# A linear-attention round in a new order: next k turned beside the scores, outputs in the middle, state at the end

## The reference

```python
for t in range(S):
    cur = np.einsum('bhd,bhe->bhde', u[None] * kt, vt)
    y[:, :, t] = np.einsum('bhd,bhde->bhe', rt, state + cur)
    state = wt[:, :, :, None] * state + np.einsum('bhd,bhe->bhde', kt, vt)
```

## Time and profile before

| | us |
|---|---|
| median of 3 runs | 448.57 |
| lowest and highest of them | 442.07, 450.49 |
| the profiled execution | 442.72 |
| its span in the trace | 441.2 |
| TensorE busy | 409.9 (93%) |
| VectorE busy | 215.4 (49%) |
| GpSimd busy | 167.2 (38%) |
| ScalarE busy | 110.5 (25%) |

### The profile page before, as it was taken

The page is one execution under the profiler, slowest core; times in us unless marked ns, Lnnn a source line. Parts: engine busy times, 40 slices in busy tenths (PEclk is TensorE's granted clock), DMA queues, the critical chain, the costliest instruction groups (busy, mean ns, idle before and its releaser), DMA issues.

```text
span 441.2 us, 6924 instructions
## 1 busy us (share of the span) xinstructions
PE 409.9 (93%) x2682; PEld 394.6 (89%) x2682; DVE 215.4 (49%) x416; ACT 110.5 (25%) x218; POOL 167.2 (38%) x174
## 2 busy tenths in 40 slices
PE   5459898798998999999999999999999999999997
PEld 5448787687888989998999999999999999999997
DVE  4077788679876985623165365635013203212311
ACT  3244244334451110204730021224013103201300
POOL 6173647445424783434769999200000000000000
PEclk9957699789999999999999999999999999999999
DMA  9965443244442310020021233000010000000000
GB/s 141 273 121 124 104 106 84 41 104 99 117 91 36 91 37 0 1 73 0 2 72 37 72 107 108 3 0 1 18 37 0 19 18 19 2 36 18 1 19 36
DMA packets 60130, 25.04 MB, mean 57 GB/s; under 512 B 51136, under 2 KB 58176, under 8 KB 60096
## 3 DMA queue, kind: packets, MB, share of 16 engines
q1 hardware_dynamic: 60096, 24.58, 23.8%
HBM read 22.22 MB, written 2.36 MB: 56 GB/s over the span
## 4 chain that ended last, share of the span: by engine, by line
PE 77%; DVE 10%; issue 6%; SPq 3%; POOL 2%; DMA 2%; ACT 0%; DVEq 0%; POOLq 0%
PE bank L1020 21%; PE bank L1022 21%; PE bank L1021 21%; PE bank L1107 5%; PE bank L1103 2%; DVE suf L796 2%; DVE pre L805 2%; DVE am L829 2%; DMA ub<-in_u 2%; PE bank L1070 2%; SPq L332 1%; PE bank L1140 1%; PE bank L1158 1%; PE bank L1034 1%; POOL rp L525 1%
## 5 line engine op out<-in xcount | busy, mean ns | idle before, releaser
L716 ACT ACTIVATE ha_hi<-bank 128x384 fp32r<-128x384 f32 x48 | 23.6, 492 | 113.1 <-PE bank L1022 113.1
L941 DVE SCALAR_TENSOR_TENSOR ha_lo<-bank,ha_hi 128x384 fp32r<-128x384 f32 x48 | 26.8, 558 | 50.2 <-ACT ha_hi L716 50.2
L1020 PE MATMUL bank<-c_hi,ha_lo 128*128 128x384 f32 x144 | 48.2, 335 | 0.0
L1022 PE MATMUL bank<-c_hi,ha_hi 128*128 128x384 f32 x144 | 48.1, 334 | 0.0
L1022 PE MATMUL bank<-u2T_hi,c_hi 128*128 128x384 f32 x144 | 48.1, 334 | 0.0
L1021 PE MATMUL bank<-c_lo,ha_hi 128*128 128x384 f32 x144 | 48.1, 334 | 0.0
L1020 PE MATMUL bank<-u2T_hi,c_lo 128*128 128x384 f32 x144 | 48.1, 334 | 0.0
L1021 PE MATMUL bank<-u2T_lo,c_hi 128*128 128x384 f32 x144 | 48.1, 334 | 0.0
L946 DVE TENSOR_TENSOR x<-bank,x 128x384 f32<-128x384 f32 x12 | 6.7, 558 | 65.3 <-PE bank L1022 65.3
L1020 PE MATMUL bank<-sg_hi,z_lo 128*128 128x384 f32 x96 | 32.7, 341 | 1.9 <-issue 1.3
L525 POOL TENSOR_TENSOR rp<-rT,pre 112x512 f32<-112x512 f32 x12 | 15.3, 1277 | 46.6 <-ACT rT L648 41.5
(11 more groups left out here) (142 smaller groups left out, 938.1 us busy)
## 6 DMA issues: line engine op xcount, KB each, us to landing
raw<-in_moe_w_ch SPq DMA_DIRECT2D x12, 384.0 KB, 3.1
kc<-in_k SPq DMA_DIRECT2D x12, 192.0 KB, 3.2
rc<-in_r SPq DMA_DIRECT2D x12, 192.0 KB, 3.6
vn<-in_v SPq DMA_DIRECT2D x12, 192.0 KB, 2.9
raw<-in_moe_w_sg SPq DMA_DIRECT2D x6, 384.0 KB, 4.2
out<-x SPq DMA_DIRECT2D x12, 192.0 KB, 1.9
raw<-in_moe_w_in SPq DMA_DIRECT2D x4, 384.0 KB, 6.2
raw<-in_moe_w_tok SPq DMA_DIRECT2D x4, 384.0 KB, 3.4
```

The costliest lines, as they stand in the source:

```text
L716: sc.activation(ha[0][:, i, :], bank[:, 0:HALF], ACT.Relu).then_inc(act_out, 1)
L941: ve.scalar_tensor_tensor(ha[1][:, i, :], bank[:, 0:HALF], 0.0, ha[0][:, i, :].bitcast(F32), ALU.max, ALU.subtract).then_inc(dve_out, 1)
L1020: te.matmul(dst, left[1], right[0], start=first, stop=False)
L1022: return te.matmul(dst, left[0], right[0], start=False, stop=last)
```

## The change

The rounds are put in another order on TensorE and VectorE, and the jobs are dealt anew to the slots.

- TensorE: turn_w(1) stands ahead of the first scores. In a round: scores, kp turned, next k turned, slot 0, next r turned, outputs, w of n + 2 turned, range sum (round 2), slot 1, state products, slot 2. The next k waits for the state sum of the round before, the state products for the next round's kp. Eight calls of the filler matmul go (`keep_busy(4)` in slot 1 of rounds 0 and 1).
- VectorE: decays of n + 1, masks, slot 0, k scaled for n + 1, y and x of the same round, slot 1, state, diagonal of n + 1, slot 2. `st` is made by four `tensor_scalar`, one for each pair of heads, in place of one `tensor_tensor`. The range is marked and counted in round 2.
- ScalarE: the state is copied behind the jobs of slot 2, and the range checks are spread over rounds 0 and 1.
- GpSimd: the products of round 1, a weight split and chunk 2 without its `diagonal_v` come ahead of the branch. The splits of `w_out` are a round later.
- SyncE: k(1) and u are issued ahead of v(0) and r(1). v waits for the state products too. Some weight pieces come a round later.

```diff
 SLOT = {
-    (2, 2): [("xT", 0, 0), ("xT", 0, 1)],
-    (3, 0): [("v", 0, 0)], (3, 1): [("xT", 0, 2)], (3, 2): [("v", 0, 1)],
-    (4, 0): [("v", 0, 2)], (4, 1): [("xT", 0, 3)], (4, 2): [("u", 0, 0), ("wsg", 0, 0), ("wsg", 0, 1)],
-    (5, 0): [("v", 0, 3)], (5, 1): [("xT", 0, 4)], (5, 2): [("u", 0, 2), ("wsg", 0, 2), ("wsg", 0, 3)],
-    (6, 0): [("v", 0, 4)], (6, 1): [("xT", 0, 5), ("u", 0, 4)], (6, 2): [("wsg", 0, i) for i in range(4, 8)],
-    (7, 0): [("v", 0, 5)], (7, 1): [("u", 0, 6), ("u", 0, 1)], (7, 2): [("wsg", 0, 8), ("u", 0, 3), ("wsg", 0, 9)],
-    (8, 0): [("u", 0, 5), ("wsg", 0, 10)], (8, 1): [("u", 0, 7), ("wsg", 0, 11)], (8, 2): [("sg", 0, 0)],
-    (9, 0): [("sg", 0, 1)], (9, 2): [("sg", 0, 2)],
-    (10, 0): [("sg", 0, 3)], (10, 2): [("sg", 0, 4)],
-    (11, 0): [("sg", 0, 5)], (11, 2): [("sg", 0, 6)],
+    (3, 0): [("xT", 0, 0), ("xT", 0, 1)], (3, 1): [("xT", 0, 2)], (3, 2): [("v", 0, 0), ("u", 0, 0)],
+    (4, 0): [("xT", 0, 3)], (4, 1): [("v", 0, 1)], (4, 2): [("u", 0, 2), ("v", 0, 2)],
+    (5, 0): [("v", 0, 3)], (5, 1): [("xT", 0, 4), ("u", 0, 4)], (5, 2): [("wsg", 0, 0), ("wsg", 0, 1)],
+    (6, 0): [("v", 0, 4)], (6, 1): [("xT", 0, 5), ("u", 0, 6)], (6, 2): [("wsg", 0, 2), ("wsg", 0, 3)],
+    (7, 0): [("v", 0, 5), ("u", 0, 1)], (7, 1): [("u", 0, 3)], (7, 2): [("wsg", 0, i) for i in range(4, 8)],
+    (8, 0): [("u", 0, 5), ("wsg", 0, 8), ("wsg", 0, 9)], (8, 1): [("u", 0, 7)],
+    (8, 2): [("wsg", 0, 10), ("wsg", 0, 11)],
+    (9, 0): [("sg", 0, 0)], (9, 2): [("sg", 0, 1)],
+    (10, 0): [("sg", 0, 2)], (10, 1): [("sg", 0, 3)], (10, 2): [("sg", 0, 4)],
+    (11, 0): [("sg", 0, 5)], (11, 1): [("sg", 0, 6)],
 }
...
                     sp.wait_ge(av_done, n - VR + 1)
+                    sp.wait_ge(ds_done, states(n - VR))
                     sp.wait_ge(base_done, n - VR + 1)
...
             load_w(1)
+            load_k(1)
+            sp.dma_start(ub[:, :], u.rearrange("(a h) d -> a (h d)", a=1).to_broadcast([PART, C])).then_inc(ub_in, 16)
             load_v(0)
             load_r(1)
-            load_k(1)
...
-            sp.dma_start(ub[:, :], u.rearrange("(a h) d -> a (h d)", a=1).to_broadcast([PART, C])).then_inc(ub_in, 16)
...
-                diagonal_v(n)
+                if n != 2:
+                    diagonal_v(n)
...
                 gp.tensor_copy(flag[:, :], nhalf[:, :]).then_inc(flagged, 1)
-                chunk_products(1)
-                for n in range(2, NCH):
+                diagonal_v(2)
+                chunk_products(2)
+                for n in range(3, NCH):
...
             chunk(1)
+            chunk_products(1)
+            chunk(2)
             pool.wait_ge(ok_counted, 1)
...
-                ve.tensor_tensor(st[0:QP, :, :], su[0:QP, :, :], suf[0:QP, :, 0:1].to_broadcast([QP, NP, D]), ALU.mult
-                                 ).then_inc(st_done, 1)
+                for p in range(NP):
+                    ins = ve.tensor_scalar(st[0:QP, p, :], su[0:QP, p, :], suf[0:QP, p, 0:1], None, ALU.mult)
+                ins.then_inc(st_done, 1)
...
             for n in range(NCH):
-                if n:
-                    y_tile(n - 1)
-                    if n > 2:
-                        x_tile(n - 1)
                 if n + 1 < NCH:
                     decays(n + 1)
+                if n == 0:
+                    diagonal(0)
+                mask(n, 0)
+                mask(n, 1)
                 if n == 2:
+                    mark_range()
+                take_slot(n, 0)
+                if n + 1 < NCH:
+                    scale_k(n + 1)
+                if n == 2:
+                    count_range()
                     x_tile(0)
                     x_tile(1)
-                if n == 1:
-                    mark_range()
-                take_slot(n, 0)
+                y_tile(n)
+                if n >= 2:
+                    x_tile(n)
+                take_slot(n, 1)
                 if n % NC < NC - 1:
                     state(n)
-                mask(n, 0)
-                mask(n, 1)
-                take_slot(n, 1)
-                if n == 1:
-                    count_range()
                 if n + 1 < NCH:
-                    scale_k(n + 1)
                     diagonal(n + 1)
                 take_slot(n, 2)
...
                 if n:
                     pe.wait_ge(kp_done, n)
-                    pe.wait_ge(su_done, states(n - 1))
+                if n >= 2:
+                    pe.wait_ge(su_done, states(n - 2))
...
-                pe.wait_ge(kp_done, n + 1)
+                pe.wait_ge(kp_done, n + 2)
...
             keep_busy(8)
+            turn_w(1)
             for n in range(NCH):
                 scores(n)
                 turn_kp(n)
-                if n == 0:
-                    turn_w(1)
+                if n + 1 < NCH:
+                    turn_k(n + 1)
                 if n < 3:
                     keep_busy(4)
                 for job in slot_jobs(n, 0):
                     product(*job)
                 if n + 1 < NCH:
                     turn_r(n + 1)
+                outputs(n)
+                if n + 2 < NCH:
+                    turn_w(n + 2)
+                if n == 2:
+                    sum_range()
+                for job in slot_jobs(n, 1):
+                    product(*job)
                 if n % NC < NC - 1:
                     state_products(n)
-                for job in slot_jobs(n, 1):
-                    product(*job)
-                if n < 2:
-                    keep_busy(4)
-                if n == 1:
-                    sum_range()
-                if n + 2 < NCH:
-                    turn_w(n + 2)
-                if n + 1 < NCH:
-                    turn_k(n + 1)
                 for job in slot_jobs(n, 2):
                     product(*job)
-                outputs(n)
```

More of the change, by code:

```diff
@@ L381, in _ @@
             load_v(2)
-            later = {1: [3], 2: [4], 3: [5], 4: [6], 5: [7], 6: [8], 7: [9, 10], 8: [11], 9: [12], 10: [13], 11: [14]}
+            later = {1: [3], 2: [4], 3: [5], 4: [6], 6: [7], 7: [8], 8: [9, 10], 9: [11], 10: [12], 11: [13, 14]}
             for n in range(1, NCH):
@@ L564, in split_gated @@
                                  ).then_inc(g_split, 1)
-            early = {0: [("w_in", 2)], 1: [("w_in", 3)], 2: [("w_in", 0)], 3: [("w_in", 1)], 8: [("w_out", 0)],
-                     9: [("w_out", 1)]}
+            early = {0: [("w_in", 2)], 1: [("w_in", 3)], 2: [("w_in", 0)], 3: [("w_in", 1)], 9: [("w_out", 0)],
+                     10: [("w_out", 1)]}
             def chunk(n):
@@ L754, in _ @@
                     take_job(*job)
+                if n == 0:
+                    check_range(4)
+                    check_range(5)
+                for job in slot_jobs(n, 2):
+                    take_job(*job)
                 if n % NC < NC - 1:
@@ L757, in _ @@
                 if n == 0:
-                    for i in range(4, CHECKS):
-                        check_range(i)
-                for job in slot_jobs(n, 2):
-                    take_job(*job)
+                    check_range(6)
+                    check_range(7)
+                if n == 1:
+                    check_range(8)
+                    check_range(9)
                 for s in range(3):
@@ L964, in _ @@
             scale_k(0)
-            diagonal(0)
             for n in range(NCH):
-                if n:
-                    y_tile(n - 1)
-                    if n > 2:
-                        x_tile(n - 1)
                 if n + 1 < NCH:
                     decays(n + 1)
+                if n == 0:
+                    diagonal(0)
+                mask(n, 0)
+                mask(n, 1)
                 if n == 2:
+                    mark_range()
[4 more added lines that the diff above has]
+                    count_range()
                     x_tile(0)
                     x_tile(1)
-                if n == 1:
-                    mark_range()
-                take_slot(n, 0)
+                y_tile(n)
+                if n >= 2:
+                    x_tile(n)
+                take_slot(n, 1)
                 if n % NC < NC - 1:
                     state(n)
-                mask(n, 0)
-                mask(n, 1)
-                take_slot(n, 1)
-                if n == 1:
-                    count_range()
                 if n + 1 < NCH:
-                    scale_k(n + 1)
                     diagonal(n + 1)
@@ L993, in _ @@
                             mean_shift(b, i)
-            y_tile(NCH - 1)
-            x_tile(NCH - 1)
             for kind, b, i in TAIL:
```

## The result

| | before | changed |
|---|---|---|
| median | 447.28 us | 448.10 us |
| lowest to highest | 441.83 to 450.49 | 447.25 to 450.69 |
| profiled span | 441.2 us | 446.7 us |
| mean granted clock of the span | 0.960 | 0.943 |

The changed kernel takes 1.0089 times as long as before, with a 95% interval of 1.0058 to 1.0121: 0.9% slower, and 0.2% by the medians of the table, where 436 us were forecast and 427 to 446 given as the range. The times of the kernel before spread over 9 us, as its clock does; its median was 447.7, 444.3 and 445.5 us in the three sets of runs behind the experiments. The ratios are taken within a set, over those runs of each kernel that lie within 1.5% of its fastest one, which are two of six for the kernel with u early alone. Where medians and ratios give different prices, both are named; a price by a ratio is worked out with 444 us for the kernel before.

What follows compares the result with a forecast made beforehand. All gain or loss lies ahead of TensorE's fixed tail at 179.5 us, chiefly the decays stall. Tail from 166.8 plus 4.2 for one clock fall is 171.0, 8.5 earlier: 434.2, plus 2 for gaps, 436 us; range 427 to 446.

Steps and rivals of the forecast that it cites:

- Early u: Round 0: u lands near 10 us instead of 20.84, so scores(1) run from 17.8 instead of 33.0; 15 us won.
- The walk: Rounds 0 to 11 followed chain by chain: outputs(3) end at 56.7 us, tail from 166.8 before the charged clock fall.
- The wait of turn_k for k(2): Ahead of outputs(1): k(2) still lands at 24.9 us, TensorE idles 5.5 us and loses its clock, assumed half for 7 us.
- The waits for the masks: Outputs wait for VectorE's masks in rounds 3, 4, 5 and 8; 3.7 us at least ahead of outputs(3).
- The chain of VectorE that sets rounds 3 to 5: y, x, state, dg, decays and masks: 6.9 us from the outputs' end, plus VectorE's slot jobs and any state wait.
- The clock: One fall charged at outputs(3) and the work behind, 4.2 us, plus 2 us for other gaps.
- rival C: Gaps of VectorE's chain (4 to 5, 5 to 6, 7 to 8) cost the clock repeatedly, 5 us each: 451; chance 0.10.
- Both signs of being wrong: Wrong if the clock stays below full beyond 62 us, or the range check's verdict comes later than 44 us.
- Eight filler matmul calls fewer: they ran in waits: TensorE's dropped filler calls, priced at nothing because they ran in waits.
- st at 0.5 us: VectorE's state step: four tensor_scalars taken at 0.5 us, bounds 0.45 and 3.8, since dg, of one SBUF source, was never held.
- Rival B: The four st's are held as the one was, 1.5 us in five gaps, 7.5 us: 443; chance 0.17.

Runs made afterwards that it cites:

- new order, filled: The changed kernel with filler matmuls (identity times itself, into a free bank) in TensorE's waits of rounds 1 to 5: 432.53 us, ratio 0.9704.

## Why the prediction was wrong, step by step

**Early u: right.** Scores(1) forecast at 17.8 us, measured 18.04. The wait for the decays is gone. The edit alone is worth 9 us in the old order by the medians; the forecast of a faster kernel rested on this step, and the step holds.

**The walk: right in its chains, and its sum in part by luck.** With no fall but the one in the wait for k(2), which it walked at half clock for an assumed 7 us, it summed to 430.0 us for the execution; the new order with the clock held up takes 432.5. Against that run, its scores(2) came 3.1 us late and its outputs(3) 0.9, while what follows was 3.4 us too short (tail start less outputs(3) end, 110.1 against 113.5). Its parts (us):

| | forecast, no fall but for k(2) | changed | new order, filled |
|---|---|---|---|
| scores(2) start | 33.5 | 31.92 | 30.37 |
| kn(2) ready | 38.7 | 38.2 | |
| flag | 44.4 | 46.7 | |
| outputs(3) end | 56.7 | 62.35 | 55.8 |
| outputs(3) to outputs(4) | 10.9 | 13.1 | 11.6 |
| outputs(4) to outputs(5) | 14.1 | 16.3 | 15.1 |
| outputs(5) to outputs(6) | 9.0 | 11.3 | 9.3 |
| tail start | 166.8 | 185.0 | 169.3 |

The wait of turn_k for k(2) was named at 5 to 6 us near 19 to 25 and measured 5.05 us up to 24.79. The waits for the masks are the largest in rounds 3, 4 and 5, as named (2.38, 1.70 and 1.70 us); round 6 has one of 1.05 that wasn't named, and the one named in round 8 is 0.43. The chain of VectorE that sets rounds 3 to 5 was the right one.

**The clock: the step that failed.** "I charge one fall: ... 4.2", and 2 us more for the gaps. Beside the one for k(2) three falls came, at 38.3, 75.8 and 96.4 us. From the walk without them to the measured tail there are 185.0 - 166.8 = 18.2 us: outputs(3) end 5.65 later, of which the flag is 2.3 (outputs(2) and the range sum ran at half clock ahead of it) and outputs(3) at half clock 5.1 - 2.7 = 2.4 (0.9 of the 5.65 aren't assigned, a held st of 1.87 us at 50.44 among them); the three gaps behind are 2.2, 2.2 and 2.3 longer; outputs(4) and (5) take 4.7 and 5.1 instead of 2.7; the later gaps add 1.4 in all. The fillers show that it is the clock: with them 15.6 us come back. The terms charged 6.2. This is rival C's mechanism, but only one of its three places: the fall at 96.4 ends the gap 4 to 5; those that it puts in 5 to 6 and 7 to 8 didn't come (outputs(6) and (8) ran at full clock behind waits of 1.05 and 0.43 us), and two came that it didn't name, in round 2 and at the end of 3 to 4. That C's price of 451 is near 448.1 is luck as far as its places go. Both signs of being wrong that the prediction set came true: the clock was below full beyond 62 us, and the verdict of the range check came later than 44 us (VectorE's count ends at 46.3 us, the flag is set at 46.7). C had a chance of 0.10, and the argument against it was the flaw: one idle of 1.3 us near 135 us, behind which the clock stayed full, was taken for the rule. That idle is almost the only one about: between 126 and 142 us of the kernel before TensorE is busy 14.7 of 16.0. In rounds 3 to 5 of the changed kernel it is busy 23.04 us of 27.3, 7.00 of 10.2 and 10.77 of 13.9 in the rows above, with several idles each, and there waits of 1.7 us were followed by falls. The nearer row was at hand: the earlier trace rows had round 4 of the kernel before at 13.7 busy of 18.4 us and 0.88 of the clock.

Also too small was the length of a fall. The price took 7 to 10 us of half clock for each; the one at 38.3 us lasted 27.3 us. At half clock the whole span loses 15.6 us for 50.5 us, 0.31 us for each, less than the 0.5 of a TensorE that is never idle, and the likely reason, not tested by itself, is that TensorE's waits for VectorE's chain hide part of it.

**"Eight filler matmul calls fewer: they ran in waits", at nothing: open, and doubtful.** The changed kernel lost fillers and opened a wait of 5.05 us where one of 9.8 had been. Fillers in rounds 1 and 2 bring 4.0 us. They are 34 calls against the eight that the change drops, and those eight alone weren't put back, so their share isn't measured, and that it cost nothing isn't shown either way.

**st at 0.5 us: wrong in its reason, small in its effect here.** Free, four take 0.71 us (18.99 in the timeline), not 0.5. Beside GpSimd's work they take 1.85 and 1.87 us, as the earlier trace rows had the one at a median of 1.87. The reason given was that dg, of one SBUF source, was never held; it doesn't carry over to a tensor_scalar. The Trainium skill's rule as the prediction quoted it ("VectorE: DVE Perf Modes", Mode 2×_2P, with "GPSIMD Engine Reference", Specifications), that a tensor_scalar of fp32 in SBUF takes both ports, speaks for the held rows, and the trace agrees with it. Rival B had the mechanism, but its price of 7.5 us didn't come: the changed kernel's forty last 10.3 us in all, 1.03 for each state where 0.5 were put into the chain, as only three of the ten states are held; and with one st the filled kernel is within what the runs can tell.

**k(2): right as a wait; its worth stays open.** The prediction names it as the new wait and builds the rest of round 1 on it, which is right by the rows. In the filled kernel TensorE still waits 1.0 us for it, and the clock that fell in this wait makes scores(2) 1.5 us later (31.92 against 30.37). With k(2) early scores(2) begin at 30.37 either way, but there the later check_w took its place.

**What the old order still has over the new.** With fillers and the same single st, in one set of runs, 431.13 against 427.88: 3.2 us. Without fillers and with four st's, 9.8 or more. So by the medians 5.2 to 6.6 of the 9.8 us are the clock, half to two thirds, the four st's are at most 1.4, and 3.2 are the order with its deal and its checks. Which wait makes these 3.2 stays open: moving the checks or k(2) and the old deal in the new order won nothing, but each of these runs lost clock elsewhere as well.

## What to carry to other kernels

A wait in a TensorE-bound stream costs itself and the clock behind it: judge a new order by all its idles, round by round, against rounds of the trace that look alike, and where several lie close together, count the stretch behind them at half clock (7 to 27 us here) or fill the waits with matmuls into a free bank, which brought 15.6 us to one order and, by the medians, 8 to 10 to the other. Make the one edit that the stall asks for by itself first: issuing u early, without the reordering, brought 2 to 3%, and with fillers 3.4%; and look beside which GpSimd instructions a short VectorE operation falls before it is split into several.

## What the runs showed of the hardware

- Half clock with TensorE busy 84%: 23.04 of 27.30 us at 0.50. Two stretches in which it was busy less (7.00 of 10.20, 10.77 of 13.90) had the full clock.
- The same work of TensorE up to 27 us, with an idle time of 5.0 us in it, had the clock fall at 21.3 us and return at 28.1 in one run, and fall at 23.8 and return at 40.9 in another, whose 17.1 us at 0.50 had TensorE busy for 16.15.
- Waits of 1.70 us, in rounds 4 and 5, were followed by falls within 0.4 us. In the filled kernel one wait of the same 1.7 us cost no clock.
- A tensor_scalar with an fp32 tensor in SBUF (112x48) is held by GpSimd like a tensor_tensor of two: 0.71 us for four, 1.85 and 1.87 beside its work. Several of four short ones in a row can be held anew: 1.66, 0.88, 0.23 and 1.81 us, 4.33 in all, across four GpSimd instructions, where one tensor_tensor of the same 112x192 took 1.83.
